# An attention phase with two feed-forward blocks behind it: the decay tables' products, the state sums and the copies of outputs in another order in the first steps

## What is computed

```
scores = scale * np.matmul(q, k.transpose(0, 1, 3, 2))
gamma = 1.0 - 2.0 ** (-5.0 - np.arange(H, dtype=np.float32))
Dmat = np.where(rel >= 0, gamma[:, None, None] ** rel[None, :, :], 0.0)
ret = scores * Dmat[None, :, :, :]
return np.matmul(ret, v).astype(np.float32)
...
h = np.maximum(np.maximum(x @ w1, x @ w2), x @ w3)
return (h @ w_out).astype(np.float32)
...
a = x @ w1
b = x @ w2
h = a * b @ w3
return (h @ w_out).astype(np.float32)
```

## Time and profile before

| | |
|---|---|
| median of 3 runs | 1230.52 us (1230.19 to 1233.7) |
| profiled execution | 1231.16 us |
| its span | 1229.3 us |
| TensorE busy | 1219.6 us (99%) |
| VectorE, ScalarE, GpSimd busy | 736.0, 486.4, 434.1 us |

### The profile page before, as it was taken

The page is one execution under the profiler, slowest core; times in us unless marked ns, Lnnn a source line. Parts: engine busy times, 40 slices in busy tenths (PEclk is TensorE's granted clock), DMA queues, the critical chain, the costliest instruction groups (busy, mean ns, idle before and its releaser), DMA issues.

```text
span 1229.3 us, 21619 instructions
## 1 busy us (share of the span) xinstructions
PE 1219.6 (99%) x8572; PEld 1200.2 (98%) x8572; DVE 736.0 (60%) x1065; ACT 486.4 (40%) x781; POOL 434.1 (35%) x234
## 2 busy tenths in 40 slices
PE   8999999999999999999999999999999999999999
PEld 7899999999999999999999999999999999999998
DVE  5555648845545464658787777453545356786553
ACT  3433544423223232326555544232323244554441
POOL 3535628220200102052967661202020216466550
DMA  9999944120203011053465441313131342444441
GB/s 343 331 334 351 338 136 147 46 84 33 97 26 101 29 63 67 26 174 137 151 223 191 157 158 55 104 52 109 53 110 58 109 168 108 154 155 161 159 157 65
DMA packets 87332, 169.55 MB, mean 138 GB/s; under 512 B 9272, under 2 KB 58680, under 8 KB 87232
## 3 DMA queue, kind: packets, MB, share of 16 engines
q1 hardware_dynamic: 87232, 168.17, 38.9%
HBM read 106.27 MB, written 61.87 MB: 137 GB/s over the span
## 4 chain that ended last, share of the span: by engine, by line
PE 96%; DMA 1%; DVE 1%; issue 1%; ACT 0%; SPq 0%; ACTq 0%; DVEq 0%
PE ps L1246 28%; PE ps L1248 28%; PE ps L1247 28%; PE ps L1162 3%; PE ps L1109 2%; PE ps L1150 2%; PE ps L1177 1%; PE ps L1132 1%; PE ps L1181 1%; PE ps L1179 1%; DMA hd<-h 1%; DVE probs L943 0%; PE ps L1114 0%; DMA pows<-powers 0%; DMA raw<-hd 0%
## 5 line engine op out<-in xcount | busy, mean ns | idle before, releaser
L1246 PE MATMUL ps<-chi,whi 128*128 128x384 f32 x2016 | 674.1, 334 | 1.3 <-ACT w L922 0.7
L1248 PE MATMUL ps<-chi,wlo 128*128 128x384 f32 x2016 | 673.4, 334 | 0.0
L1247 PE MATMUL ps<-clo,whi 128*128 128x384 f32 x2016 | 673.4, 334 | 0.0
L668 POOL TENSOR_TENSOR raw<-raw,raw 128x768 f32<-128x768 f32 (+3 forms) x102 | 270.4, 2671 | 581.5 <-DMA raw<-xd 203.7
L1246 PEld LDWEIGHTS ps<-chi,whi 128*128 128x128 f32 x2016 | 378.4, 188 | 3.1 <-issue 1.0
L1247 PEld LDWEIGHTS ps<-clo,whi 128*128 128x128 f32 x2016 | 378.5, 188 | 0.0
L1248 PEld LDWEIGHTS ps<-chi,wlo 128*128 128x128 f32 x2016 | 378.4, 188 | 0.0
L931 DVE TENSOR_TENSOR clo<-raw,chi 128x768 fp32r<-128x768 f32 (+2 forms) x168 | 254.7, 1544 | 34.4 <-ACT chi L846 34.4
L846 ACT CAST chi<-raw 128x768 fp32r<-128x768 f32 (+2 forms) x168 | 180.2, 1081 | 84.3 <-PE ps L1248 50.5
L922 ACT COPY w<-ps 128x384 f32<-128x384 f32 x126 | 60.5, 480 | 240.0 <-PE ps L1248 238.5
L909 ACT COPY u<-ps 128x384 f32<-128x384 f32 x126 | 60.7, 482 | 160.6 <-PE ps L1248 159.0
(11 more groups left out here) (61 smaller groups left out, 814.0 us busy)
## 6 DMA issues: line engine op xcount, KB each, us to landing
gd<-h SPq DMA_DIRECT2D x96, 192.0 KB, 1.9
raw<-gd SPq DMA_DIRECT2D x24, 768.0 KB, 6.1
qks<-qk SPq DMA_DIRECT2D x30, 576.0 KB, 7.4
hd<-h SPq DMA_DIRECT2D x72, 192.0 KB, 1.9
raw<-hd SPq DMA_DIRECT2D x24, 576.0 KB, 6.0
x2d<-h SPq DMA_DIRECT2D x48, 192.0 KB, 2.9
raw<-x2d SPq DMA_DIRECT2D x24, 384.0 KB, 4.5
outT<-h SPq DMA_DIRECT2D x48, 192.0 KB, 1.9
```

Source lines behind the costliest of these rows:

```text
L668: return nc.gpsimd.tensor_tensor(out_, a, b, op)
L1246: nc.tensor.matmul(to, w1, x1, start=(start and k == 0), stop=False, skip_group_check=True)
L1247: nc.tensor.matmul(to, w1, x2, start=False, stop=False, skip_group_check=True)
L1248: last = nc.tensor.matmul(to, w2, x1, start=False, stop=(k == KH[st] - 1), skip_group_check=True)
```

## The change

Five edits, all in the order of instructions.

1. Step 0. The DMA of pows is issued second. `decay_powers` stands behind the scores of pair 0, into bank S_WC, `mask_decay` ahead of the first state; `query_powers` stands behind the scores of pair 1, waiting for dec. The state sum of pair 1 uses the bank S_STATE; the two idle products there are removed.
2. Step 2. The state sums of pairs 4 and 5 stand ahead of the queries; `make_state` of these pairs waits for the queries that read the old state.
3. Step 4. ScalarE copies the outputs of pairs 6 and 7 and scales the values of pairs 10 and 11 ahead of the copy of the folded block.
4. ScalarE splits uo block 3 in step 3, ahead of the scaling of pairs 8 and 9, not in step 4; GpSimd its low part at the end of step 3.
5. SyncE, in its part for step 2: values of pairs 8 and 9 ahead of uo block 2, and the keys of pairs 8 and 9, which wait for state sums, ahead of uo block 3 and the tails.

```diff
+SUMS_FIRST = (4, 5)
...
-UO_SPLIT = {2: 0, 3: 1, 4: 3}
+UO_SPLIT = {2: 0, 3: 1}
...
             load_qk(0)
+            sp.wait_ge(pows_zeroed, 1)
+            sp.dma_start(pows[0:HEADS, :], powers).then_inc(pows_loaded, 16)
             load_decay(0)
...
-            sp.wait_ge(pows_zeroed, 1)
-            sp.dma_start(pows[0:HEADS, :], powers).then_inc(pows_loaded, 16)
...
-                if m in (2, 3):
-                    for n in made_in(m + 1):
+                if m == 2:
+                    for n in made_in(3):
                         load_k(n)
...
-                if m == 2:
-                    load_uo(2)
-                    load_uo(3)
...
                 if 2 * m + 4 < NP:
                     load_two_v(m + 2)
+                if m == 2:
+                    load_uo(2)
+                    for n in made_in(4):
+                        load_k(n)
+                    load_uo(3)
...
-                if m in WC_READ:
+                if m in WC_READ and not late_quarters(m):
                     read_wc(WC_READ[m])
                 for n in read_in(m):
                     read_values(n)
                 if m == 3:
                     split_uo(2)
+                    split_uo(3)
                 for n in made_in(m + 1):
                     decay_values(n)
+                if m in WC_READ and late_quarters(m):
+                    read_wc(WC_READ[m])
...
             def make_state(n):
...
+                if n in SUMS_FIRST:
+                    dve.wait_ge(queried, n - 1)
...
                     if n == 0:
                         pe.wait_ge(pows_loaded, 16)
+                        decay_powers()
+                        sum_state(0)
+                    if n == 1:
+                        pe.wait_ge(dec_made, 1)
                         query_powers()
-                        sum_state(0)
-                        run_idle(2, 2)
-                    if n == 1:
                         pe.wait_ge(state_made, NC)
-                        decay_powers()
-                        pe.wait_ge(qtab_made, 1)
                         sum_state(1)
                 for i in quarters(m):
                     wc_quarter(i)
+                for n in made_in(m):
+                    if n in SUMS_FIRST:
+                        sum_state(n)
                 for n in read_in(m):
                     query_state(n)
                 for n in made_in(m) if m else ():
-                    sum_state(n)
+                    if n not in SUMS_FIRST:
+                        sum_state(n)
```

More of the change, by code:

```diff
@@ L748, in _ @@
             for m in range(STEPS - 1):
-                if m == 4:
-                    split_uo(3)
                 if m in U3_SPLIT:
@@ L958, in make_state @@
                 p = n % PAIRS
-                bank = S_WC if n == 1 else S_STATE
                 dve.wait_ge(state_summed, n + 2 - n % 2 if n >= 2 else n + 1)
+                if n in SUMS_FIRST:
+                    dve.wait_ge(queried, n - 1)
                 for c in range(NC):
-                    new = ps[:, bank, (n % 2 * NC + c) * DH:(n % 2 * NC + c + 1) * DH]
+                    new = ps[:, S_STATE, (n % 2 * NC + c) * DH:(n % 2 * NC + c + 1) * DH]
                     if c == 0:
@@ L976, in mask_decay @@
                     dec[:, 1, :, :, :].rearrange("p n h c -> p (n h) c"),
-                    ps[:, S_STATE, :].rearrange("p (n c) -> p n c", c=CH),
+                    ps[:, S_WC, :].rearrange("p (n c) -> p n c", c=CH),
                     mask.unsqueeze(1).broadcast_to([P, 4, CH]), ALU.mult).then_inc(dec_made, 1)
@@ L1006, in _ @@
                     if n == 0:
+                        mask_decay()
                         make_state(n)
@@ L1009, in _ @@
                     decay_tail(n)
-                if m == 0:
-                    mask_decay()
                 if m in P1_W_LO:
@@ L1119, in sum_state @@
             def sum_state(n):
-                bank = S_WC if n == 1 else S_STATE
                 pe.wait_ge(v_decayed, 2 * n + 2)
                 pe.wait_ge(k_loaded[keys_sem(n)], keys_count(n))
-                if n == 2:
-                    pe.wait_ge(dec_made, 1)
                 if n >= 2:
@@ L1131, in sum_state @@
                         at_ = (n % 2 * NC + c) * DH
-                        last = nc.tensor.matmul(ps[own, bank, at_:at_ + DH],
+                        last = nc.tensor.matmul(ps[own, S_STATE, at_:at_ + DH],
                                                 keys_of(n)[:, keys:keys + DH], vdec[n % 2][:, c, own],
@@ L1170, in wc_quarter @@
                     pe.wait_ge(u3_lo, kb + 1)
+                    if kb == 0:
+                        pe.wait_ge(qtab_made, 1)
                     if kb:
@@ L1195, in decay_powers @@
                     for h in range(2):
-                        last = nc.tensor.matmul(ps[:, S_STATE, (2 * n + h) * CH:(2 * n + h + 1) * CH],
+                        last = nc.tensor.matmul(ps[:, S_WC, (2 * n + h) * CH:(2 * n + h + 1) * CH],
                                                 pows[:, h * P:(h + 1) * P],
```

## The result

The changed kernel took 1233.38 us (median of 17 executions, 1230.76 to 1236.24), the kernel before beside it 1231.36 us (17 executions, 1229.98 to 1233.7). The ratio is 1.0017, 95% interval 1.0009 to 1.0025: slower by about 2 us. Forecast were 1230.3 us, range 1228.2 to 1231.6, and a shift of -0.2 us. The range did not hold the time. Of the 3.1 us between forecast and median, 0.84 is the reference: the three runs that I started from had a median of 1230.52, and seventeen have 1231.36. The rest is a real loss that I didn't forecast.

The account below looks back on a forecast made before the run. TensorE bounds the kernel nearly throughout, so shifts in steps 0 to 4 stay. Terms +0.43 - 1.24 + 1.97 - 1.36 = -0.2 us take 1231.16 to 1230.96; the median, 0.64 lower, gives 1230.3 us, range 1228.2 to 1231.6.

Parts of the forecast that it names:

- a shift of -0.2 us: Whole kernel: the sum of the terms for steps 0, 2 and 4, +0.43 - 1.24 + 1.97 - 1.36 us.
- against 51.96 that is -0.18 us: Start of step 5's scores: forecast at 51.78 us, set against 51.96 in the profile of the kernel before.
- Step 0: Probabilities of pair 2 start at 15.55 us, a loss of +0.43 us, bounds +0.2 and +0.85.
- my 4.6: Step 0 as changed: scores of pair 1 at 9.65 us, scores of pair 2 at 14.25 us.
- a gain of 0.6 at the scores of pair 1: Step 0: these scores start at 9.65 us instead of 10.20, when their rows land.
- The second term: Step 0: loads behind pows are issued some tenths of a microsecond later; costed at nothing because the queue is full.
- Step 2: Sums, queries and values run without a wait, ending at 29.41 us: a gain of 1.24 us by itself.
- Step 4: Uo block 3 lands at 43.5 us, TensorE waits 2.0 us for scaled values, step 5's scores start at 51.78.
- rival 3: Step 0: TensorE falls to the lower clock, some +2 us there, end moved by 0 to +0.5; chance 0.05.
- step 4 swallows a fall in step 0: Step 4: its wait of 2.0 us absorbs a clock loss from step 0, so the end moves by 0 to +0.5.

Follow-up runs that it names:

- e7_uo3_alone: Kernel before with only uo block 3's split moved to step 3 and the queue's new order: 1233.43 against 1231.20 us, ratio 1.0015.
- e8_best: Changed kernel, both powers in step 0's first hole, split of uo block 3 behind the scaling: 1232.60 against 1231.20 us, ratio 1.0009.
- e10_best2: Changed kernel, both powers and idle products in first hole, uo block 3 split behind scaling, folded block's copy earlier: 1230.03 against 1231.18 us, ratio 0.9990.
- e5_again: Changed kernel again, one blank line more: 1232.30 us against 1231.20 for the kernel before, ratio 1.0014.
- copies 1 to 3: Changed kernel, unaltered, run again for more profiles: 1230.52, 1231.87 and 1230.57 us, against 1230.37 for the kernel before.
- e3_without_step0: Changed kernel with step 0 as in the kernel before: 1232.08 against 1231.85 us, ratio 1.0001.
- e11_before_filled: Kernel before with 4 idle products in its wait for pows in step 0: 1230.71 against 1231.18 us, ratio 0.9994.
- e2_step0_alone: Kernel before with the edits of step 0 alone: 1232.33 against 1231.85 us, ratio 1.0002.
- e6_uo3_behind: Changed kernel with ScalarE's split of uo block 3 behind the scaling of pairs 8 and 9: 1232.05 against 1231.20 us, ratio 1.0008.
- the four copies: Changed kernel, unaltered, run four more times for profiles: 1230.52, 1231.87, 1230.57 and 1232.83 us, against 1230.37 for the kernel before.
- e4_both_in_hole: Kernel before with step 0 as changed, but both powers in the first hole, queries' first: 1231.73 against 1231.85 us, ratio 1.0002.
- copy 1: Changed kernel, unaltered, first of four further runs for profiles: 1230.52 us, against 1230.37 for the kernel before.
- e9_before_again: Kernel before again, one blank line more: 1231.71 against 1231.18 us, ratio 0.9999.
- copy 2: Changed kernel, unaltered, second of four further runs for profiles: 1231.87 us, against 1230.37 for the kernel before.
- e1_fill: Changed kernel with 5 and 4 idle products in the two waits of step 0: 1232.08 against 1231.85 us, ratio 1.0001.
- e12_fill_uo3: Changed kernel, idle products in both waits of step 0, split of uo block 3 behind the scaling: 1230.61 against 1231.18 us, ratio 0.9993.
- copy 4: Changed kernel, unaltered, last of four further runs for profiles: 1232.83 us, against 1230.37 for the kernel before.

## Why the prediction was wrong

**What bounds the kernel.** Right: the time is TensorE's, and the shift of a single execution is decided before step 5; the last column of the table stays within 1 us of 1177.3, and of the experiments that aren't in it e7_uo3_alone, e8_best and e10_best2 lie outside (1179.4, 1179.2 and 1179.3).

**The step that failed** is the comparison that ends the sum, "against 51.96 that is -0.18 us", and with it the chance of 0.05 for the clock. The forecast course of the changed kernel came true at full clock (e5_again and copies 1 to 3): the scores of pair 2, the landing of uo block 3 and the scores of step 5 stand within 0.6 us of it. But it was set against the rows of one execution of the kernel before. At the scores of pair 1 these are late by 0.5 to 0.8 us against three other profiles with step 0 in its old order, and at step 5 by 1.1 us against the one of them that has the other steps unchanged too; and the clock was taken to hold because it had held behind one wait. What the runs showed in its place is a loss of 1.33 us at full clock and one of 0.5 by more falls, worked out below.

**Step 0.** +0.43 us was forecast. The mechanism, the scaling of pair 1 behind qtab's copy behind the query powers, is there (profile of the changed kernel, 12 to 15.3 us). Two things are mis-sized. In every profile with the clock at 1.00 throughout step 0 the scores of pair 2 start 3.35 us behind those of pair 1 with step 0 as before (13.55 less 10.20; 12.72 less 9.37 in e3_without_step0; 13.01 less 9.66 in e7_uo3_alone; 12.85 less 9.50 in e11_before_filled), and 4.53 us with step 0 as changed (14.10 less 9.57 in e5_again, and the same in e2_step0_alone, e6_uo3_behind and the four copies). The rows of e11_before_filled, then those of e5_again:

```profile
9.50 1.16 PE L1109 MATMUL ps<-qks_first 64*128 64x128 f32 x16
...
12.85 1.16 PE L1109 MATMUL ps<-qks 64*128 64x128 f32 x16 [0.31 <-DVE probs L952]
```

```profile
9.57 1.16 PE L1118 MATMUL ps<-qks_first 64*128 64x128 f32 x16 [0.74 <-DMA qks_first<-qk]
...
14.10 1.16 PE L1118 MATMUL ps<-qks 64*128 64x128 f32 x16
```

So the order costs 1.18 us, as my 4.6 had it; 1.0 of it is left at the scores of pair 4, 12.52 us behind those of pair 1 instead of 11.52. What I set against it was a gain of 0.6 at the scores of pair 1, from 10.20 to 9.65. The 9.65 was right (9.57, 9.70, 9.82, 9.84 and once 8.83), but 10.20 was late: pows landed at 7.89 us there, and the other three have it at 7.06 to 7.19 and these scores at 9.37 to 9.66. The gain isn't there, and e2_step0_alone has +1.0 us in the time at full clock, though its interval (0.2 to 1.9) reaches down to the 0.43. The second term is SP's later issue, which I costed at nothing because a full queue lands by bytes. It is nothing in e5_again and the copies, where the first state sum starts at 7.64 to 8.14 and waits 0 to 1.0 us, and not in the first profile, e4_both_in_hole and e8_best, where it waits 2.0, 1.5 and 1.6 us for keys issued some 0.75 us later than before. Those three are the ones whose clock then fell in step 0. What sets them apart, though, is less the keys, issued at 3.35 us in all of them, than the first scores: there they took 1.16 or 1.17 us and ended early, and in the other profiles with edit 1, but for copy 1, 1.5 to 2.1.

**Step 2.** Right in the order: sums, queries, values without a wait, 7.3 us from the scores of pair 4 to those of pair 6 in e5_again (22.09 to 29.36). The gain of 1.24 was too large: the profile of before took 8.37, 1.10 more, and e9_before_again, e11_before_filled and e4_both_in_hole took 7.99, 0.72 more. In e6_uo3_behind and copy 2 TensorE stood still for 1.0 and 0.7 us ahead of the last product of the queries, and the profile names nobody that it waited for; there the gain isn't left.

**Step 4.** Right to 0.6 us at full clock: landing 43.5, step 5 at 51.78, against 43.1 to 44.1 and 51.4 to 52.3 (e5_again and the first three copies). That the end is tied to this landing is shown by the table, and that the place of ScalarE's split in edit 4 is the cause by the pairs e1_fill and e12_fill_uo3 (-1.6 us) and e5_again and e6_uo3_behind (-1.0), each at full clock. But the sum compared this end with 51.96, again the one row of before. Where its step 0 runs without a long wait for pows, step 5 starts at about 51 us (50.86 in e11_before_filled), and against that the same landing is a loss of 1 us and not a gain of 0.2. This reading rests on e11_before_filled and the rows above; no second profile of the kernel before at full clock is on record, and by its time the first isn't late (1231.16 us, where the 66 take 1231.06 in the mean). It is the other profiles that lie below the mean of their sets (e2_step0_alone 1230.32 to 1232.12, e11_before_filled 1229.84 to 1230.67, e5_again 1231.57 to 1232.10).

**The clock.** I gave rival 3 a chance of 0.05 and named against it one wait of 1.29 us that was followed by full pace. That was one execution of a kernel that falls in 39 of 105. In the changed kernel 16 of 28 timed executions fell (by chance alone, at the rate of the kernel before, that or more would come about in 5 of 100 cases), at a mean of 1234.3 us against 1232.4 for the other 12. The changed kernel has more places for it: up to 2.0 and 1.5 us of wait in step 0, and 0.4 to 3.2 us in step 4. In which of them the timed executions fell isn't on record: of the profiles of this kernel one fell in step 0 and one, copy 4, in step 4. The rival had the size about right in the mean (1.9 us for a fall, where it had 2) and the place, and was wrong in holding that step 4 swallows a fall in step 0: in the first profile the state sums of pair 6, for which SP waits ahead of the keys of pair 8, started at 39.28 us and not at 35.01 as in e5_again, SP issued uo block 3 at 40.86 instead of 36.59, and step 5 started 3.2 us later. The trace agrees with the rule in the Trainium skill (TensorE: Matmul & The Clock Gate, "What's actually happening") that activity holds the clock up and idleness throttles it, and the idle products in the hole are the test of it: 11 of 11 at full clock in e11_before_filled, 9 of 12 in e1_fill and 10 of 12 in e12_fill_uo3, against 12 of 28 in the changed kernel.

**How the 2 us are made up,** from the executions' means: all of before 1231.67 (105), the changed kernel 1233.47 (28), a difference of 1.8. At full clock the difference is 1.33 (1232.39 against 1231.06; 0.7 to 2.0). I put that down to step 0's order and the wait behind uo block 3: each has about its size in an experiment of its own, but all with intervals of 0.6 to 1 us each way, and the full-clock profiles of the changed kernel (1230.52 to 1231.87 us) lie below its full-clock mean, so a part of it may stand where no profile shows it. The remaining 0.5 is the clock: falls in 57% instead of 37%, each at 1.9 instead of 1.6 us. The clock is what I had all but ruled out, but not the larger part. What stays open: why the first loads land up to a microsecond earlier or later between executions of one kernel (pows at 7.06 to 7.89 with its issue in its old place), what lengthens the way of uo block 3, and when the long wait for wlo in a later stage comes.

## What to carry to other kernels

One profile is one draw. Where a term of some tenths of a microsecond is taken from a wait that ends in a load, take it from several executions, and look at the mean clock of all of them before calling a hole harmless. A load split moved ahead of other work on an in-order engine ties that work to the load's landing: here it cost 1.0 to 1.6 us at full clock. And a hole in front of TensorE early in a kernel is worth filling with products that nobody reads before any reordering is tried: here that alone made the falls go (11 of 11 at full clock) and the median 0.5 us lower, which isn't clear of noise, where filling and the best reordering together gave 1.15, which is.

## What was not expected of the hardware

The granted clock fell to 0.50 behind waits of 2.0 and 0.6 us, 1.5 and 0.7, 1.6 and 0.7, 2.2 (in e9_before_again, and again in e7_uo3_alone at 583 us) and 3.2 us, and within one of 3.9 us. It did not behind one of 1.3 us in my first profile, nor behind 1.0 and 1.3 us in step 0 of copy 1, nor behind 1.5 and 1.5 us in that of copy 2, which is what fell elsewhere, nor behind the 2.0 us in step 4 of copy 1, nor behind 2.2 us at 580 us in e10_best2. So the length of a wait alone doesn't decide it in these runs, and what does stays open. One thing goes with it in step 0: the four profiles with a fall there all have the first scores at the fast pace (1.16 or 1.17 us), which of the other fourteen only copy 1 has. The clock came back after 3.5 us in one case (before again, 7.8 to 11.3 us) and after 10.2 us in another (10.7 to 20.9 us, with a 1.5 us wait inside). In e11_before_filled 1.16 us of idle products, with 0.25 us of wait left behind them, kept it up.

The first scores take 1.16 us in some executions, 2.08 in others and something between in the rest, with the granted clock at 1.00 in all (the earlier trace rows and before again, from 4.34 us, are the two ends). The faster pace doesn't help: the next work waits for the same load, and the hole in which the clock falls is longer by as much.
